# Later 1/rms chunks from block rows, a one-copy fp32 Gram, and an expert quarter in the token array's place

## What is computed

```python
# attention over queries pooled in pairs: 576 rows per batch, 8 heads
q_pool = q.reshape(B, H, S // 2, 2, D).mean(axis=3)
attn = softmax(q_pool @ k.T / sqrt(D))
x = (attn @ v) as (4 * 576, 512)              # 2304 tokens
# soft mixture of experts, 32 slots
logits = x @ phi
d = softmax(logits, over tokens)              # dispatch
slot_input = d.T @ x                          # 32 x 512
slot_out[e] = relu(slot_input[e] @ w1[e]) @ w2[e]    # 512 -> 1024 -> 512
c = softmax(logits, over slots)               # combine
x = c @ slot_out
# gated layer with RMS norm
xn = x / sqrt(mean(x * x) + 1e-6) * rms_g
return (silu(xn @ w_gate) * (xn @ w_val)) @ w_out    # 512 -> 1536 -> 512
```

## Time and profile before

| | |
|---|---|
| median of three runs | 841.78 us |
| profiled execution, time | 841.03 us |
| profiled execution, span | 839.0 us |
| TensorE matmul, busy | 794.5 us, 95% |
| TensorE weight loads, busy | 603.3 us, 72% |
| VectorE, busy | 497.7 us, 59% |
| ScalarE, busy | 461.7 us, 55% |
| GpSimd, busy | 171.3 us, 20% |
| DMA, mean over the span | 136 GB/s |
| granted TensorE clock, whole span | 1.00 |

### The profile page before, as it was taken

How to read it: one execution, slowest core, us unless ns; L and a number is a source line. 1 busy time by engine, 2 the same in 40 slices (tenths; PEclk the granted TensorE clock), 3 DMA queues, 4 the chain that set the end, 5 groups by cost and what they waited for, 6 DMA issues and landing times. The chain is left out here.

```text
span 839.0 us, 17251 instructions
## 1 busy us (share of the span) xinstructions
PE 794.5 (95%) x5738; PEld 603.3 (72%) x5738; DVE 497.7 (59%) x958; ACT 461.7 (55%) x888; POOL 171.3 (20%) x230
## 2 busy tenths in 40 slices
PE   1799999999999999999999999998889999999997
PEld 1677777777777777787777777764334788888875
DVE  3466576666666766666766657646311566666664
ACT  1467666667666666676666766642112554343342
POOL 1323314224133142241341430000000340000000
PEclk9999999999999999999999999999999999999999
DMA  8993473553744735637438326737899201010111
GB/s 217 281 210 85 115 170 79 149 118 93 183 95 102 190 73 131 143 80 171 106 91 197 77 64 162 281 105 251 327 388 408 80 1 51 0 52 6 45 51 26
DMA packets 86329, 114.40 MB, mean 136 GB/s; under 512 B 48144, under 2 KB 50192, under 8 KB 85776
## 3 DMA queue, kind: packets, MB, share of 16 engines
q1 hardware_dynamic: 85488, 112.68, 47.9%
q10 hardware_dynamic: 800, 1.18, 0.7%
HBM read 71.37 MB, written 4.72 MB: 91 GB/s over the span
## 5 line engine op out<-in xcount | busy, mean ns | idle before, releaser
L490 PE MATMUL scores<-k_stack,q_stack 128*128 128x384 f32 x960 | 276.3, 378 | 15.9 <-DMA q_stack<-q_lo 15.3
L438 PE MATMUL tbank<-ident,probs 128*128 128x128 f32 x1296 | 220.0, 279 | 2.8 <-DVE pt L737 2.4
L639 ACT COPY pt<-tbank 128x384 f32<-128x384 f32 x256 | 122.7, 479 | 142.9 <-PE tbank L438 141.7
L438 PEld LDWEIGHTS tbank<-ident,probs 128*128 128x128 f32 x1296 | 156.6, 140 | 59.3 <-issue 42.7
L611 ACT ACTIVATE probs<-scores,neg_max 128x1152 f32<-128x1152 f32 x144 | 175.8, 1221 | 24.5 <-DVE neg_max L686 17.9
L490 PEld LDWEIGHTS scores<-k_stack,q_stack 128*128 128x128 f32 x960 | 148.8, 192 | 17.7 <-DMA q_stack<-q_lo 16.4
L682 DVE TENSOR_REDUCE row_max<-scores 128x1 f32<-128x384 f32 x144 | 80.1, 556 | 130.1 <-PE scores L490 128.3
L525 PE MATMUL obank<-pt,v_in 128*64 128x256 f32 x1152 | 148.8, 389 | 0.0
L675 DVE TENSOR_REDUCE row_max<-scores 128x1 f32<-128x768 f32 x144 | 136.8, 950 | 16.3 <-PE scores L490 13.5
L525 PEld LDWEIGHTS obank<-pt,v_in 128*64 128x64 f32 x1152 | 72.8, 136 | 49.3 <-issue 23.5
L323 POOL TENSOR_TENSOR k_hi<-k_lo,one 128x512 fp32r<-128x512 f32 (+1 forms) x45 | 37.2, 826 | 304.0 <-ACT k_lo L567 283.2
(11 more groups left out here) (169 smaller groups left out, 752.3 us busy)
## 6 DMA issues: line engine op xcount, KB each, us to landing
weights<-in_moe_w SPq DMA_DIRECT2D x7, 2048.0 KB, 11.1
k_in<-in_k SPq DMA_DIRECT2D x32, 288.0 KB, 4.7
v_in<-in_v SPq DMA_DIRECT2D x16, 576.0 KB, 4.0
k_stack<-k_hi SPq DMA_DIRECT2D x31, 288.0 KB, 4.0
k_stack<-k_lo SPq DMA_DIRECT2D x31, 288.0 KB, 3.5
q_in<-in_q SPq DMA_DIRECT2D x16, 512.0 KB, 4.9
slots_of_four<-in_moe_w SPq DMA_DIRECT2D x3, 2048.0 KB, 12.1
weights<-in_moe_w SPq DMA_DIRECT2D x12, 512.0 KB, 11.2
```

Of the source, the lines that this page charges most:

```text
L438: last = nc.tensor.transpose(tbank[:, bank, cols], src, ident[0:rows, 0:rows])
L490: last = nc.tensor.matmul(scores[:, bank, 0:CH], q_stack[at.par][:, h, order, cols], k_stack[at.par][:, h, keys], start=(x == 0), stop=(x ...
L639: nc.scalar.copy(pt_out(at, e), tbank[:, bank_of(at, e), 0:3 * P].rearrange("p (r q) -> p r q", r=3)).then_inc(out_by_act, 1)
```

## The change

Three things are changed.

- *An expert quarter.* w1 quarter 1 of the second group goes to `w1_second`, in the place of `x_nat`, and is issued in the dispatch block once `z_ready` is there. Quarters 2 and 3 take chunks 0 and 1 of the lower slots, w2 quarters 0 and 1 chunks 2 and 3, w2 quarters 2 and 3 slots 4 and 5. `w1_second` shares its place with `comb_cat` and `plain_t`, so VectorE's `split_comb` moves to group 1, after two of its w1 quarters have been used. `keep_clock` gets 4 and 8 tiles instead of 12 and 12.
- *The Gram.* `st_plain` is one copy instead of four; the Gram's four rows of blocks come from four column groups, all in fp32; VectorE masks it with `high_mask`, and ACT has no part in it. `keep_clock` before and after it gets 1 and 1 tiles instead of 4 and 2.
- *1/rms.* Chunk 0 is broadcast as before. For the others `tok_a` is transposed (20 x 128), VectorE spreads it over block rows `rows` (20 x 768), ACT makes `rows_hi`, VectorE `rows_lo`, and each chunk is two fp32r matmuls. ACT's order changes: rows_hi and inverse_out(0) come ahead of the Silu table, and h_hi(0) ahead of inverse_out(3).

```diff
+    w1_second = mem.sb("w1_second", [P, 4, F1], FP32)
+    mem.at -= SLOT
     comb_cat = mem.sb("comb_cat", [P, NI * B, 4, NS], F32R)
...
+    w1_next = [w1_first[:, :, :], w1_second[:, :, :], upper[:, :, 0, :], upper[:, :, 1, :]]
+    w2_next = [upper[:, :, 2, :], upper[:, :, 3, :]] + [mem.slots[n]... for n in (4, 5)]
...
         sp.dma_start(w1_next[0], ...).then_inc(w1_in[0], 16)
+        sp.wait_ge(z_ready, 1)
+        sp.dma_start(w1_next[1], ...).then_inc(w1_in[1], 16)
...
-        for c in range(1, KT):
-            sp.wait_ge(w1_used, c)
+        for c in range(2, KT):
+            sp.wait_ge(w1_used, c - 1)
             sp.dma_start(w1_next[c], ...).then_inc(w1_in[c], 16)
         for n in range(4):
             if n == 0:
+                sp.wait_ge(w1_used, KT - 1)
+            elif n == 1:
                 sp.wait_ge(h_ready, 2)
             else:
                 sp.wait_ge(o_ready, 1)
...
-                        keep_clock(12)
+                        keep_clock(2 * f - 4)
...
+        def broadcast_first():
+            for t in range(NF):
+                last = nc.tensor.matmul(banks[:, INV_BANK[0], P * t:P * t + P],
+                                        tok_a[:, B * t:B * t + 1].broadcast_to([P, P]), ident[:],
+                                        start=True, stop=True)
+            last.then_inc(bcast_ready, 1)
+
         def broadcast_inverse(n):
...
+            pe.wait_ge(rows_step, 4)
+            first, width = (0, N) if n < B else (N, TAIL * B)
+            out_bank = banks[:, INV_BANK[n], 0:width]
+            pick = row_batch[:, n:n + 1].broadcast_to([NI * B, P])
+            nc.tensor.matmul(out_bank, pick, rows_hi[:, first:first + width], start=True, stop=False)
+            nc.tensor.matmul(out_bank, pick, rows_lo[:, first:first + width], start=False, stop=True
+                             ).then_inc(bcast_ready, 1)
...
-        keep_clock(4)
-        pe.wait_ge(st_out, NG + 1)
+        keep_clock(1)
+        pe.wait_ge(st_out, NG)
         for c in range(KT):
-            last = nc.tensor.matmul(g_ps, st_plain[:, c, :, :].rearrange("p a s -> p (a s)"), st_plain[:, c, 0, :],
-                                    start=(c == 0), stop=(c == KT - 1))
+            for j in range(4):
+                last = nc.tensor.matmul(g_ps[32 * j:32 * j + 32, :], st_plain[:, c, :], st_plain[:, c, :],
+                                        start=(c == 0), stop=(c == KT - 1), tile_position=(0, 32 * j))
...
-        pe.wait_ge(gram_step, 2)
+        pe.wait_ge(gram_step, 1)
...
         pe.wait_ge(inv_ready, 1)
-        broadcast_inverse(0)
+        nc.tensor.transpose(rows_ps, tok_a[:], ident[:]).then_inc(rows_ready, 1)
+        broadcast_first()
...
-        act.wait_ge(gram_ready, 1)
-        nc.scalar.copy(gram_hi[:], g_ps).then_inc(gram_step, 1)
...
         high_half(0)
+        act.wait_ge(rows_step, 2)
+        nc.scalar.copy(rows_hi[:], rows[:]).then_inc(rows_step, 1)
+        inverse_out(0)
         nc.scalar.activation(warm[:, 1:2], ident[:, 0:1], ACT.Silu)
-        inverse_out(0)
...
-                if k == 0:
-                    inverse_out(3)
                 act.wait_ge(hid_done, k + 1)
                 halves_free(n, f)
                 nc.scalar.copy(h_hi[...], hid2[...]).then_inc(hi_done, 1)
                 if k == 0:
+                    inverse_out(3)
                     share_out(7)
                     inverse_out(4)
...
-        split_comb(dve)
-        build_spread()
+        build_spread(dve)
         for g in range(NG):
+            if g:
+                dve.wait_ge(w1_used, KT + 1)
+                split_comb(dve)
...
-            for rep in range(4):
-                last = nc.vector.tensor_copy(st_plain[:, :, rep, 16 * g:16 * g + 16]..., st_ps...)
+            nc.vector.tensor_copy(st_plain[:, :, 16 * g:16 * g + 16]..., st_ps...).then_inc(st_out, 1)
...
+        dve.wait_ge(gram_ready, 1)
+        nc.vector.tensor_scalar(gram[:], g_ps, high_mask[:, 0:1], None, ALU.mult).then_inc(gram_step, 1)
...
+        dve.wait_ge(rows_ready, 1)
+        nc.vector.tensor_tensor(rows[:, 0:N]..., rows_ps..., row_tile..., ALU.mult).then_inc(rows_step, 1)
+        nc.vector.tensor_tensor(rows[:, N:]..., rows_ps..., ident..., ALU.mult).then_inc(rows_step, 1)
         low_half(0)
         share_out(0)
+        dve.wait_ge(rows_step, 3)
+        nc.vector.tensor_tensor(rows_lo[:], rows[:], rows_hi[:].bitcast(FP32), ALU.subtract).then_inc(rows_step, 1)
         share_out(2)
```

More of the change, by code:

```diff
@@ L781, in rest @@
     assert mem.at >= loads_end
-    upper = mem.slots_of_four[:, :, :, :]
-    w1_next = [w1_first[:, :, :]] + [upper[:, :, c, :] for c in range(3)]
-    w2_next = [upper[:, :, 3, :]] + [mem.slots[n][:, :].rearrange("p (r n) -> p r n", r=4) for n in (4, 5, 6)]
     w2_last_in = sem("w2_last_in")
@@ L815, in rest @@
     spread = mem.sb("spread", [P, 2, 4, 4, NS], F32R)
-    gram_hi = mem.sb("gram_hi", [P, NS], F32R)
-    gram = mem.sb("gram", [P, NS], F32R)
+    gram = mem.sb("gram", [P, NS], FP32)
     comb_t = mem.sb("comb_t", [P, SQ], FP32)
@@ L820, in rest @@
     row_group = mem.sb("row_group", [P, B], FP32)
+    row_tile = mem.sb("row_tile", [NI * B, NI], FP32)
+    row_batch = mem.sb("row_batch", [NI * B, B + 1], F32R)
+    batch_sum = mem.sb("batch_sum", [NI * B, B], FP32)
     tail_inv = mem.sb("tail_inv", [P, B // 2], FP32)
@@ L823, in rest @@
     assert mem.at <= mem.x_end
+    upper = mem.slots_of_four[:, :, :, :]
+    w1_next = [w1_first[:, :, :], w1_second[:, :, :], upper[:, :, 0, :], upper[:, :, 1, :]]
+    w2_next = [upper[:, :, 2, :], upper[:, :, 3, :]] + [mem.slots[n][:, :].rearrange("p (r n) -> p r n", r=4) for n in (4, 5)]
     def tile_cols(b, i):
@@ L1055, in build_spread @@
         nc.vector.memset(product[:, SQ:], 0.0)
+        cells = ident[0:NI * B, 0:NI * B].rearrange("p (i b) -> p i b", b=B)
+        nc.vector.tensor_reduce(row_tile[:], cells, axis=AX.X, op=ALU.add)
+        nc.vector.tensor_reduce(batch_sum[:], cells.rearrange("p i b -> p b i"), axis=AX.X, op=ALU.add).then_inc(cat_step, 1)
+        dve.wait_ge(cat_step, 1)
+        nc.vector.tensor_copy(row_batch[:, 0:B], batch_sum[:])
+        nc.vector.tensor_scalar(row_batch[:, B:B + 1], batch_sum[:, 0:1], 0.0, 1.0, ALU.mult, ALU.add)
         nc.vector.memset(eps[:], 1e-6)
@@ L1066, in rest @@
     w_lo = mem.sb("w_lo", [P, 2, QW], F32R)
+    rows_lo = mem.sb("rows_lo", [NI * B, N + TAIL * B], F32R)
     assert mem.at <= r2 + 2 * SLOT
+    mem.at = r2 + 2 * SLOT + 4 * NFT * DM
+    rows = mem.sb("rows", [NI * B, N + TAIL * B], FP32)
+    rows_hi = mem.sb("rows_hi", [NI * B, N + TAIL * B], F32R)
+    assert mem.at <= r2 + 4 * SLOT
     mem.at = r2 + 4 * SLOT
@@ L1086, in rest @@
     sq_ps = banks[:, 1, 0:NI * B]
+    rows_ps = banks[0:NI * B, 3, 0:P]
     w_ps = banks[:, 4:6, :]
@@ L1267, in stack_share @@
                              w_lo[:, m, :], start=False, stop=True).then_inc(wl_ready, 1)
-        def broadcast_inverse(n):
-            out_bank = banks[:, INV_BANK[n], :]
-            if n < B:
-                for t in range(NF):
-                    last = nc.tensor.matmul(out_bank[:, P * t:P * t + P],
-                                            tok_a[:, B * t + n:B * t + n + 1].broadcast_to([P, P]), ident[:],
-                                            start=True, stop=True)
-            else:
-                for b in range(B):
-                    last = nc.tensor.matmul(out_bank[:, TAIL * b:TAIL * b + TAIL],
-                                            tok_a[0:TAIL, B * NF + b:B * NF + b + 1].broadcast_to([TAIL, P]),
-                                            ident[0:TAIL, 0:TAIL], start=True, stop=True)
-            last.then_inc(bcast_ready, 1)
+        def broadcast_first():
[4 more added lines that the diff above has]
+            last.then_inc(bcast_ready, 1)
+        def broadcast_inverse(n):
+            pe.wait_ge(rows_step, 4)
[5 more added lines that the diff above has]
+                             ).then_inc(bcast_ready, 1)
         def gate(n, f):
@@ L1304, in _ @@
             for b in range(B):
-                last = nc.tensor.matmul(yt_ps[32 * b:32 * b + 32, bank, 0:width], gram[:].bitcast(FP32),
+                last = nc.tensor.matmul(yt_ps[32 * b:32 * b + 32, bank, 0:width], gram[:],
                                         plain_t[:, first + width * b:first + width * (b + 1)].bitcast(FP32),
@@ L1308, in _ @@
         last.then_inc(yt_ready, 1)
+        pe.wait_ge(st_out, NG + 1)
         share(0, 0)
```

41 lines of the change are left out of this document (24 added, 17 removed).

## The result

| | before | after |
|---|---|---|
| median of the runs at the first comparison | 841.78 us (5 runs, 841.15 to 843.36) | 835.95 us (5 runs, 835.32 to 839.72) |
| ratio, 95% interval | | 0.9939, 0.9913 to 0.9964 |
| profiled execution, span | 839.0 us | 833.4 us |
| granted TensorE clock over the span | 1.00 | 0.996 |

The same kernel was timed once more, beside some of the experiments: ratio **0.9968, 0.9947 to 0.9988**. Both intervals lie under 1, so the gain is real. Its size is put at 0.3 to 0.6% (the intervals allow 0.1 to 0.9%), not at the 0.7% that the two medians alone suggest. The forecast, -0.57%, lies between. Where it comes from is the question that the traces answer better than the times.

The account below looks back on a forecast made before the run. Weight transfers, not TensorE, were taken to set the end of the stretch between the attention and last GLU loops. Gains of 3.86+0.9+0 = 4.8 us made the profiled 841.03 us 836.2, the median 837.0 (-0.57%); range 834.7 to 839.2.

Parts of the forecast that it names:

- Part 1: Expert stage: second w1 quarter issued early into the token array's place; 3.86 us gained, all of it kept.
- so the hole closes ... each lands 3.86 us earlier: Idle DMA time over 588 to 594 us vanishes, so all seven 2 MB pieces behind land 3.86 us earlier.
- TensorE's room: Second group: quarters' matmuls start at 621.75, 624.46, 629.42 after a 1.4 us wait; TensorE's own limit is 628.0.
- Part 2: Gram stage: one copy gains 0.73 us, matmuls nothing, ACT's hop 0.30; sum 1.0, taken as 0.9 us.
- the price of the 32 small records: Gram matmuls: 0.03 us each by L525's row, 0.95 together against 0.97 now, so nothing gained.
- The upper bound named in the forecast, four groups side by side: Gram stage: 1.5 us gained if four column groups run fully side by side.
- The tenth taken off for the change into the tiled mode and back: Gram stage: the sum of 1.0 us reduced to 0.9 us for entering and leaving that mode.
- Part 3: 1/rms broadcasts: 2.5 us less TensorE work, but the chain goes through ACT and VectorE; net 0 us.
- Can the value weights become the bound? No: Ahead of the last GLU loop: last value piece lands by 648.4, used about 2.5 us later, brought nearer by only 0.9.
- Rival E: Shrunken fillers and a 1.4 us wait ahead of the last quarter drop the clock for 8 us; 844.3 us, 4%.
- signs of being wrong: DMA hole left, last quarter by DMA after 630.5, clock under 1.00, 32 Gram records over 1.5 us, ACT's table load in chain.
- over 588 to 592 ... stays 1.00: Evidence against a clock fall: TensorE waited over 1 us twice there, yet the granted clock stayed 1.00.

Follow-up runs that it names:

- Issue after landing: Kernel after, with SyncE waiting for the first w1 quarter to land before it issues the second; ratio to before 0.9994, stream 56.9 us.
- scaling first: Kernel after, first two gates issued ahead of the second broadcast and scaled ahead of share_out(2); ratio to before 0.9930, run again 0.9936.
- Long fillers: Kernel after, with the fillers between the w2 quarters back at 12 and 12 tiles; ratio to before 0.9980.
- quarter only: Kernel before, with only the early second w1 quarter, split_comb moved and fillers of 4 and 8 tiles; ratio to before 0.9956.
- old broadcasts: Kernel after, without transposition, rows, rows_hi and rows_lo, all chunks by four fp32 matmuls, ACT's new order kept; ratio to before 0.9918.
- no fillers: Kernel after, with all keep_clock calls of the last block taken out; ratio to before 0.9959.
- no quarter: Kernel after, with w1 and w2 quarters, SyncE's waits and 12-tile fillers as before; ratio to before 1.0000, span 842.2 us.
- old Gram: Kernel after, with four st_plain copies, four full Gram matmuls, ACT's gram_hi and fillers of 4 and 2 tiles again; ratio to before 0.9965.
- after again: Kernel after, unchanged, timed once more beside some experiments; ratio to before 0.9968.

## Why the prediction was right, and where its sizes were off

The time, 835.95 against 837.0, and the way it came are right; the sum of 4.8 us is made of terms of which one was too large, one too small.

**Part 1 was over-sized: 3.86 us forecast, 2.4 measured.** Ten profiles have the early issue and the short fillers or none. In nine of them the last quarter waits for its weights, and in the first one stream and TensorE arrive together. There the stream takes 52.2 to 55.6 us, 53.6 in the mean, against 56.0 in the two without it. So 2.4 us in the mean, 0.4 to 3.8 from run to run. The step that failed is "so the hole closes ... each lands 3.86 us earlier". The share does close, but the rate drops at the seam, where the new piece ends and the next takes over. The windows of the repeat of the kernel after show the largest loss:

```profile
590.00:592.00 2.00, 1.63 (x8) 0.48 (x12) 1.67 (x16) 0.00 (x0) 0.00 (x0) 0.60 0.92 371
592.00:594.00 2.00, 2.00 (x16) 0.68 (x12) 0.00 (x0) 0.00 (x0) 0.00 (x0) 0.55 1.00 397
594.00:596.00 2.00, 2.00 (x24) 0.67 (x20) 0.00 (x0) 0.00 (x0) 0.00 (x0) 1.00 0.72 227
596.00:598.00 2.00, 2.00 (x24) 0.66 (x20) 0.00 (x0) 0.00 (x0) 0.00 (x0) 1.00 0.91 324
```

The hole of before has not gone altogether, it has come back later and smaller. The new piece is only one piece: it lasts 5.3 us from about 589.7, and the one behind it still waits for the first matmuls of the first group (`w1_used` 1). The forecast went through the destinations of the last pieces, but not whether the next issue comes in time behind the new one. It does so only just: 5.1 us after the new issue with the clock at 1.00, and 5.8 to 6.8 us in the six of the ten in which the clock fell there. Where it was 6.8 us the stream took 54.0, 54.4 and 55.6 us. In the four profiles at 5.1 to 5.2 us it took 52.2 to 53.8: once the whole 3.8 us was won, and in the other three up to 1.6 us were lost even then. Issue after landing lost rate at 4.5 us too. So the late issue is part of the cause, and the rest stays open.

**TensorE's room was right.** The steps 621.75, 624.46 and 629.4 describe the kernel with its clock at 1.00 and the stream at its best, and one profile has both, the first of scaling first. Less the 0.59 us by which its w2_last was issued later than before (577.91), its quarters start at 621.74, 624.65 and 629.55, the last after a wait of 1.07 us where 1.4 was forecast. Long fillers showed the other side.

**Part 2 was under-sized: 0.9 us forecast, 1.6 measured** in every profile, to 0.01 us. The step that failed is the price of the 32 small records: I took 0.03 each from two column groups (L525), so 0.95; they took 0.46 in all, 0.014 each. The upper bound named in the forecast, four groups side by side, 1.5 us, was the right one. The 62 ns for each that the Trainium skill names for matmuls that aren't decoded in hardware (TensorE: Matmul & The Clock Gate, Part 1, "Wait — 56ns, not 53.3ns?") would have given 2.0 us; the measurement decides against it here. The tenth taken off for the change into the tiled mode and back has no row of its own in any run.

**Part 3: 0 forecast, 0.45 us measured** where neither a value piece nor the clock comes in (19.30 against 18.85). The steps were right: the second broadcast waits for rows_lo, and what is lost there is regained at the end by ACT's order and the narrow broadcasts; undo either (0.40, 0.44) and the end has the length of before, so they work only together. I had set the delay in the middle somewhat too high. "Can the value weights become the bound? No" was wrong in part: in the first profile share(1,0) waited 0.21 us for its piece, and the end kept only 0.15 us of part 3; in no other profile do TensorE's matmuls wait for a value piece. I had counted the room of the last piece only, and taken it that part 2 would bring the use nearer by no more than 0.9.

**Part 3 has a price that these distances leave out.** The long fall of the clock at the loop's beginning goes with the block rows. Kernels with the old broadcasts (before, quarter only, old broadcasts) have a mean clock under 0.994 in 0 of 90 timed executions (only four of these are of the one that has part 2). Kernels with block rows in the order of the change have it in 31 of 69 (no fillers left out), without part 1 (no quarter) and without part 2 (old Gram) as well. With scaling first it is 0 of 16. TensorE is busy 10.5 of the 12 us ahead of the loop's first gate in the profiles with the old broadcasts, 9.7 to 9.8 in the two of the kernel after, where less work stands against waits as long or longer, and 10.7 with scaling first. That this is the reason is argued, not shown. In the kernel after, timed again, the five executions with the long fall take 840.8 us in the median, the other seven 838.0. So part 3 as it was built most likely costs more in time than its 0.45 us. Parts 1 and 2 alone, which would settle it, were not run.

**Rival E** happened, but elsewhere, and the forecast's sum has no term for the clock. A granted clock under 1.00 stood among its signs of being wrong, and the clock did fall in the first profile, at 590, where the evidence against it lay ("over 588 to 592 ... stays 1.00"): one profile of before, where most executions of before have a lower mean. There it hits matmuls that are ahead of the stream, but it makes the next issue later: 53.9 us of stream in the mean of the six such profiles, 53.2 in the four others. At the loop's beginning (four profiles: no quarter, old Gram, long fillers, issue after landing) it costs in full. From the sums of squares to the end of the span, no quarter takes 842.2-638.77 = 203.4 us and before 839.0-639.36 = 199.6, so 3.8 us more for about 10 us at half the clock. The forecast's price, 7.3 us for 8 us, was too high by its own terms: 8 us at half the clock hold up at most 4 us of full-clock work. Its chance, 4%, was too low: five of 17 executions of the kernel after. Over the 103 timed executions of the experiments' kernels, each against the mean of its own kernel, time and mean clock go together with a correlation of -0.74 (-0.86 to -0.93 in after again, long fillers, issue after landing and no quarter), so the falls are a good half of that spread. In the kernel before it is only -0.26 to -0.50, and most of its 5 us of spread has another cause, which stays open.

**The sum** of measured parts is 2.4+1.6+0.45 = 4.4 us, 0.53%, less the small wait where it comes in. The two comparisons gave 0.61% and 0.32%, and the first was on the lucky side: none of its five executions has the long fall of the clock, and five of the 12 in the second do. The seven without it, 838.0 against 842.99 before, give 0.59%. The forecast's 0.57% came so near because the errors of its terms, 1.5 too much in part 1 and 1.1 too little in parts 2 and 3, nearly cancel; that its time met the first median within 1.1 us owes something to luck.

## What to carry to other kernels

When an early transfer closes a hole in a stream, look at the next issue behind it as well: it may hang on an engine whose speed varies, and here the rate dropped at the seam even where it came before the piece ahead had ended. Distances between close events within one profile (here to 0.02 us) measure parts that comparisons of whole runs, 0.2% apart, can't. And after an operation is taken off one engine's queue, look for idle stretches there into which the start of the next chain can be pulled: that small reorder gave 0.9 us, twice what part 3 gave. Last, taking work off TensorE ahead of a dense stage is not free by itself: read the granted clock of every timed execution, not only that of the profiled one, before a kernel is called free of such falls.

## What was not expected of the hardware

- Small fp32 matmuls in four column groups, 32 columns each: 32 records in 0.46 us, against 8 full ones in 1.08 us.
- The granted clock fell to 0.50 in some executions around a gap of 1.4 to 1.5 us, and not in others of the same kernel (scaling first: 1.00 throughout in one profile, 0.51 at 592 to 594 in the other, after a gap of 1.48 us in both); it fell around a gap of 3.40 us where the fillers were taken out.
- The DMA engines' share can stand near 1 while the rate is a fifth to a third under the 390 to 420 GB/s of the stretches behind, around the seam between two transfers: 324 GB/s at 1.00 in the first profile after (594 to 596), 291 at 1.10 in scaling first, again (594 to 596).
